# Attention output computed feature by token, its diagonals put into the score matrix

## The reference

```
for t in range(S):
    cur = einsum('bhd,bhe->bhde', u * k[t], v[t])
    y[t] = einsum('bhd,bhde->bhe', r[t], state + cur)
    state = w[:, None] * state + einsum('bhd,bhe->bhde', k[t], v[t])
```

## Time and profile before

| what | value |
|---|---|
| median of 3 runs | 1078.55 us (1077.47 to 1079.28) |
| the profiled execution | 1079.38 us |
| its span, first to last instruction | 1077.6 us |
| mean granted TensorE clock | 0.986 of full |
| TensorE busy, weight loads busy | 1039.0 us, 1030.1 us |
| VectorE, ScalarE, GpSimd busy | 819.8, 620.1, 446.8 us |

### The profile page before, as it was taken

How to read it: one execution, slowest core, us unless ns; L and a number is a source line. 1 busy time by engine, 2 the same in 40 slices (tenths; PEclk the granted TensorE clock), 3 DMA queues, 4 the chain that set the end, 5 groups by cost and what they waited for, 6 DMA issues and landing times.

```text
span 1077.6 us, 20183 instructions
## 1 busy us (share of the span) xinstructions
PE 1039.0 (96%) x6540; PEld 1030.1 (96%) x6540; DVE 819.8 (76%) x1998; ACT 620.1 (58%) x1477; POOL 446.8 (41%) x752
## 2 busy tenths in 40 slices
PE   5779899999999999999999999999999999999998
PEld 4779899999999999999999999999999999999998
DVE  8979888877778778778777534887786777687775
ACT  4334544343344343343343366888887888788886
POOL 7878767766666767767767044000000000000000
PEclk9779999999999999999999999999999999999999
DMA  3234422121121121122212123101000000000000
GB/s 110 90 124 126 125 67 75 52 74 53 52 77 52 53 75 52 53 74 61 70 63 70 56 95 118 59 23 45 23 23 23 22 22 23 23 0 22 1 23 23
DMA packets 22016, 61.15 MB, mean 57 GB/s; under 512 B 3104, under 2 KB 9376, under 8 KB 21920
## 3 DMA queue, kind: packets, MB, share of 16 engines
q1 hardware_dynamic: 19616, 50.55, 15.4%
q10 hardware_dynamic: 2304, 9.44, 2.2%
HBM read 50.54 MB, written 9.44 MB: 56 GB/s over the span
## 4 chain that ended last, share of the span: by engine, by line
PE 77%; DVE 9%; ACT 6%; issue 4%; DMA 2%; POOL 1%; ACTq 0%; DVEq 0%; SPq 0%; POOLq 0%
PE acc L1008 31%; PE hid L992 24%; PE lev_b L1037 5%; PE lev_a L1037 5%; PE tok L1059 3%; PE lev_b L992 3%; PE lev_a L992 3%; DMA w_raw<-weights 2%; ACT scratch L919 2%; ACT scratch L918 2%; DVE scratch L749 2%; DVE scores L545 1%; PE lev_b L1031 1%; PE tok L1054 1%; DVE scratch L742 1%
## 5 line engine op out<-in xcount | busy, mean ns | idle before, releaser
L1008 PE MATMUL acc<-g_hi,w_hi 128*128 128x384 f32 x768 | 268.9, 350 | 3.8 <-ACT result L834 3.8
L1008 PE MATMUL acc<-g_hi,w_lo 128*128 128x384 f32 x768 | 258.2, 336 | 0.0
L274 POOL TENSOR_TENSOR scratch<-rk_rows,power 48x128 f32<-48x128 f32 x528 | 239.6, 486 | 42.5 <-PE lev_a L1037 39.3
L992 PE MATMUL hid<-x_hi,w_hi 128*128 128x384 f32 x576 | 193.6, 336 | 3.6 <-DVE w_lo L658 1.6
L879 ACT ACTIVATE relu_neg<-hid 128x384 f32<-128x384 f32 x128 | 62.8, 490 | 231.7 <-PE hid L992 231.3
L992 PE MATMUL hid<-x_hi,w_lo 128*128 128x384 f32 x576 | 193.0, 335 | 0.0
L1008 PE MATMUL acc<-g_lo,w_hi 128*128 128x384 f32 x768 | 174.7, 335 | 0.1
L1008 PEld LDWEIGHTS acc<-g_hi,w_hi 128*128 128x128 f32 x768 | 145.0, 189 | 6.5 <-ACT result L834 4.8
L1008 PEld LDWEIGHTS acc<-g_hi,w_lo 128*128 128x128 f32 x768 | 145.0, 189 | 0.0
L1008 PEld LDWEIGHTS acc<-g_lo,w_hi 128*128 128x128 f32 x768 | 137.2, 188 | 0.7 <-DVE g_lo L767 0.6
L664 DVE SCALAR_TENSOR_TENSOR hid<-relu_neg,neg_slope,hid 128x384 f32<-128x384 f32 x128 | 79.3, 620 | 75.1 <-ACT hid L880 74.5
(11 more groups left out here) (110 smaller groups left out, 1987.8 us busy)
## 6 DMA issues: line engine op xcount, KB each, us to landing
rkv_tok<-rkv SPq DMA_DIRECT2D x24, 576.0 KB, 4.8
w_raw<-weights SPq DMA_DIRECT2D x32, 384.0 KB, 3.1
rk_rows<-rk_t SPq DMA_DIRECT2D x48, 192.0 KB, 3.3
prev<-rkv SPq DMA_DIRECT2D x48, 192.0 KB, 4.5
x_dram<-result ACTq DMA_DIRECT2D x8, 576.0 KB, 2.8
rkv_tok<-x_dram SPq DMA_DIRECT2D x8, 576.0 KB, 3.8
out<-result ACTq DMA_DIRECT2D x8, 576.0 KB, 2.8
bonus_tok<-bonus SPq DMA_DIRECT2D x1, 192.0 KB, 6.3
```

What stands on the lines that cost most here:

```text
L274: return engine.tensor_tensor(dst, src, spread(table[rows, pairs, 0:m], 2, CHUNK // (2 * m)), ALU.mult)
L992: last = nc.tensor.matmul(to[:, 0:TILE], w[:, j, kt * P:(kt + 1) * P], x[:, par, kt], start=x is x_hi and w is w_hi and kt == 0, stop=x is ...
L1008: last = nc.tensor.matmul(acc[d][:, 0:TILE], w[:, j, cols], g[:, j % RING], start=j == 0 and g is g_hi and w is w_hi, stop=j == STEPS - 1 ...
```

## The change

- `attend` swaps the sides: state and v are the stationary operands, the scaled r and `scores` the moving ones. The output has features on partitions (a head's 48 at partition 0 or 64) and tokens in columns, one block of 128 columns of the bank per pair. The state buffer has 112 columns for it. The transposes, y_tok and the four operations of the two outside terms are gone.
- The two outside terms go into `scores`: GpSimd makes the same products (the second now with the r of the following odd token, loaded into `r_next`), VectorE's `sum_diagonal` sums them and mixes them by even and odd tokens, and `fill_diagonal` (GpSimd, once per two pairs) writes both diagonals with a mask `places`, before ScalarE and VectorE put the levels in. `scores` has a buffer for every pair.
- x_hi and x_lo are 3 blocks of 128 partitions with the features of pairs 0 to 2 on 112 of them. Pair 3 is rounded and split into `y3`, and `fill_holes` moves it by six DMAs a chunk (16 partitions, hi and lo, 128 columns) into partitions 48 to 63 and 112 to 127 of the three blocks. The first weights' rows are put into that order on the host.
- Order: the products and the sums of a chunk are made one chunk ahead, x_hi and x_lo one step earlier (the fifth step). SyncE loads a chunk with `load_chunk`: the loads, then the six small DMAs of the chunk two before it, then `r_next`. Its loop now covers six chunks. The first `up` of a tile waits for all small DMAs of the tile. In step 0 of tile 1 the score comes before the `up`.

```diff
+        x_parts = sb("x_parts", [P, 2, 2, KT, TILE], F32R)
+        x_hi, x_lo = x_parts[:, :, 0], x_parts[:, :, 1]
         g_hi = sb("g_hi", [P, RING, TILE], F32R)
         g_lo = sb("g_lo", [P, RING, TILE], F32R)
         relu_neg = sb("relu_neg", [P, 2, TILE])
...
+        scores = sb("scores", [P, PAIRS, 2, CHUNK])
+        state = sb("state", [P, 2, PAIRS, ROWS])
+        y3 = sb("y3", [P, 2, CHUNK], F32R)
         power = sb("power", [P, PAIRS, CHUNK])
         power_rev = sb("power_rev", [P, PAIRS, CHUNK])
         power_tok = sb("power_tok", [P, PAIRS, 2, D])
@@ -121,10 +122,12 @@
...
 
@@ -276,34 +281,45 @@
 
         @block.sync
         def _(sp):
-            def load_prev(c, which, done):
...
+            def load_next(c):
+
+                if isinstance(c, int):
+                    reached(sp, s_sum, c)
+                odd = rkv[bass.ds(c, 1)].rearrange("c (i b) a f -> (c i) b a f", b=2)[:, 1, 0]
+                sp.dma_start(r_next[:], spread(odd, 1, 2)).then_inc(next_in, 16)
 
             def load_rows(c, par):
 
                 if isinstance(c, int):
-                    if c >= 2:
-                        sp.wait_ge(s_sum, c - 1)
-                        load_prev(c - 1, 0, prev_k_in)
-
                     reached(sp, score_done, PAIRS * (c - 1))
                     reached(sp, rstate_done, 2 * (c - 1))
...
                     sp.dma_start(rk_rows[HALF * q:HALF * q + D, par],
                                  rk_t[bass.ds(c, 1), q].rearrange("c d a p t -> (c d) a p t")
                                  ).then_inc(rows_in[par], 16)
                 if isinstance(c, int):
-                    reached(sp, y_done, c - 1)
+                    reached(sp, av_done, PAIRS * (c - 1))
+                    reached(sp, s_next, c - 1)
                 sp.dma_start(rkv_tok[:, par], rkv[bass.ds(c, 1)].rearrange("c t a f -> (c t) a f")
                              ).then_inc(tok_in[par], 16)
-                if not isinstance(c, int):
-                    load_prev(c - 1, 0, prev_k_in)
-                if not isinstance(c, int) or c >= 2:
-                    load_prev(c - 1, 1, prev_v_in)
+
+            def fill_holes(c, odd, cc):
+
+                sp.wait_ge(xlo_done, c + 1)
+                for q in range(2):
+                    for k in range(KT):
+                        first = HALF * q + (HALF - D) * k
+                        sp.dma_start(x_parts[HALF * q + D:HALF * (q + 1), odd, :, k, cc * CHUNK:(cc + 1) * CHUNK].bitcast(F32),
+                                     y3[first:first + HALF - D].bitcast(F32)).then_inc(holes_in, 16)
+
+            def load_chunk(c, at):
+
+                load_rows(c, at % 2)
+                before = at - 2
+                fill_holes(c - 2, before // CHUNKS_PER_TILE % 2, before % CHUNKS_PER_TILE)
+                load_next(c)
 
             def load_weights(i):
                 reached(sp, wlo_done, i - 1)
@@ -311,7 +327,8 @@
 
             def load_x2(u):
...
+            with sp.Fori(1, 3) as i:
+                for at in range(8, 8 + 2 * CHUNKS_PER_TILE):
+                    load_chunk(6 * i + at - 6, at)
+            for c in range(20, CHUNKS):
...
+            def products(c, par, uses):
+
+                pool.wait_ge(tok_in[par], 16 * uses)
+                reached(pool, s_sum, c)
+                nc.gpsimd.tensor_tensor(ruk[:], rkv_tok[:, par, 0], rkv_tok[:, par, 1], ALU.mult).then_inc(s_rk, 1)
+                pool.wait_ge(s_rk, c + 1)
+                if isinstance(c, int) and c == 0:
+                    pool.wait_ge(s_small, 32)
+                nc.gpsimd.tensor_tensor(ruk[:], ruk[:], bonus_tok[:], ALU.mult).then_inc(s_ruk, 1)
+                pool.wait_ge(next_in, 16 * (c + 1))
+                nc.gpsimd.tensor_tensor(r_next[:], r_next[:], rkv_tok[:, par, 1], ALU.mult).then_inc(s_next, 1)
+
+            def fill_diagonal(c, par, x):
 
                 pool.wait_ge(s_diag, c + 1)
-                nc.gpsimd.tensor_tensor(y_tok[:, par].rearrange("p (a d) -> p a d", d=D),
-                                        rkv_tok[:, par, 2].rearrange("p (a d) -> p a d", d=D),
-                                        spread(diag[:, par], 2, D), ALU.mult)
-                pool.wait_ge(prev_v_in, 16 * (c + 1))
-                nc.gpsimd.tensor_tensor(prev[:, 1].rearrange("p (a d) -> p a d", d=D),
-                                        prev[:, 1].rearrange("p (a d) -> p a d", d=D),
-                                        spread(diag_prev[:, par], 2, D), ALU.mult).then_inc(diagv_done, 1)
+                reached(pool, av_done, PAIRS * (c - 1) + 2 * x + 2)
+                heads = 2 * PAIRS // 2
+                dst = scores[:, 2 * x:2 * x + 2].rearrange("p a h (i b) -> p (a h) i b", b=2)
+                at = spread(places[:].rearrange("p (i b) -> p i b", b=2), 1, heads)
+                value = spread(diag[:, par, heads * x:heads * (x + 1)], 2, CHUNK // 2)
+                nc.gpsimd.tensor_tensor(dst, at, value, ALU.mult).then_inc(fill_done, 1)
...
+                products(c, par, uses)
+                scale_for_state(c, par, uses)
+                fill_diagonal(c, par, 0)
                 half_of_queries(c, par, 1, not first_tile)
-                pool.wait_ge(prev_k_in, 16 * (c + 1))
-                nc.gpsimd.tensor_tensor(prev[:, 0], rkv_tok[:, par, 0], prev[:, 0], ALU.mult).then_inc(s_prev, 1)
...
                 dve.wait_ge(score_done, w + 1)
                 dve.wait_ge(high_picked, picked_through(w, rep))
                 reached(dve, state_done, w - PAIRS + 1)
-                reached(dve, av_done, w - 1)
+                reached(dve, av_done, w - PAIRS + 1)
+                dve.wait_ge(fill_done, 2 * c + p // 2 + 1)
 
                 for q in range(2):
-                    rows, cols = slice(HALF * q, HALF * q + D), slice(D * q, D * q + D)
...
@@ -550,35 +578,29 @@
             def sum_diagonal(c, par):
 
                 dve.wait_ge(s_ruk, c + 1)
-                reached(dve, diagv_done, c - 1)
-                nc.vector.tensor_reduce(diag[:, par], y_tok[:, par].rearrange("p (a d) -> p a d", d=D),
-                                        AXIS.X, ALU.add)
-                dve.wait_ge(s_prev, c + 1)
-                nc.vector.tensor_reduce(diag_prev[:, par], prev[:, 0].rearrange("p (a d) -> p a d", d=D),
+                reached(dve, fill_done, 2 * c - 2)
+                nc.vector.tensor_reduce(diag[:, par, :, 0], ruk[:].rearrange("p (a d) -> p a d", d=D),
+                                        AXIS.X, ALU.add).then_inc(s_mix, 1)
+                dve.wait_ge(s_next, c + 1)
+                nc.vector.tensor_reduce(diag_next[:], r_next[:].rearrange("p (a d) -> p a d", d=D),
                                         AXIS.X, ALU.add).then_inc(s_sum, 1)
+                dve.wait_ge(s_mix, 2 * c + 1)
+                nc.vector.tensor_scalar(diag[:, par, :, 1], diag[:, par, :, 0], odd_token[:, 0:1], None, ALU.mult
+                                        ).then_inc(s_mix, 1)
+                dve.wait_ge(s_mix, 2 * c + 2)
                 dve.wait_ge(s_sum, c + 1)
-                nc.vector.tensor_scalar(diag_prev[:, par], diag_prev[:, par], odd_token[:, 0:1], None, ALU.mult
-                                        ).then_inc(s_diag, 1)
-
-            def add_terms(c, par):
-
-                dve.wait_ge(diagv_done, c + 1)
-                nc.vector.tensor_tensor(y_tok[:, par], y_tok[:, par], prev[:, 1], ALU.add).then_inc(term_done, 1)
-
-            def add_diagonal(c, par, bank):
-
-                dve.wait_ge(term_done, c + 1)
-                dve.wait_ge(av_done, 4 * c + 4)
-                nc.vector.tensor_tensor(y_tok[:, par], bank[:, 0:FEATURES], y_tok[:, par], ALU.add
-                                        ).then_inc(y_done, 1)
+                nc.vector.scalar_tensor_tensor(diag[:, par, :, 1], diag_next[:], even_token[:, 0:1],
+                                               diag[:, par, :, 1], ALU.mult, ALU.add).then_inc(s_diag, 1)
...
-                nc.vector.tensor_tensor(x_lo[:, odd, :, columns],
-                                        bank[:, 0:FEATURES].rearrange("p (k n) -> p k n", k=KT),
-                                        x_hi[:, odd, :, columns].bitcast(F32), ALU.subtract).then_inc(xlo_done, 1)
+                nc.vector.tensor_tensor(y3[0:ROWS, 1], bank[0:ROWS, third:third + CHUNK],
+                                        y3[0:ROWS, 0].bitcast(F32), ALU.subtract)
+                nc.vector.tensor_tensor(x_lo[0:ROWS, odd, :, columns],
+                                        bank[0:ROWS, 0:third].rearrange("p (k n) -> p k n", k=KT),
+                                        x_hi[0:ROWS, odd, :, columns].bitcast(F32), ALU.subtract).then_inc(xlo_done, 1)
...
+                    last_of_chunk = rep < TILES and ends_chunk(j)
+                    following = cc + 1 < CHUNKS_PER_TILE or more
+                    opens = rep == 1 and j == 0
+                    if not opens:
+                        activate(s, j)
```

(30 more changed lines are left out.)

201 lines of the change are left out of this document (94 added, 107 removed).

## The result

The changed kernel takes 1131.34 us (median of 4 runs, 1128.66 to 1132.08), the kernel before 1078.01 in the same session: a ratio of 1.0492, 95% interval 1.0468 to 1.0516. Forecast were 1104.5 and a range of 1069 to 1126. The sign was right, the size half of what came.

The account below looks back on a forecast made before the run. TensorE was taken to bound the kernel, never resting from 151.9 to 614.7 us. Transposes -7.1, passes 0, turnovers +20, edges +11, start and tile 1 +2 gave +26 us on 1078.55: 1104.5 us, range 1069 to 1126.

Parts of the forecast that it names:

- transposes: TensorE, 21 chunks in 7 tiles: three transposes per chunk go, 0.34 us each chunk, -7.1 us.
- attend's passes: TensorE's six passes per attend stay six at unchanged cost: 0, or -9 us if two heads' passes overlap by one.
- turnovers: TensorE going to part-array products and back in each attend: 0.24 us by 84, +20 us; ends 0 and 0.70 each.
- edges, rest: TensorE waits for six small DMAs at each tile's start: about 2.0 us at five edges, 0.5 at two, +11 us.
- edges, clock: Half clock for 3 us after each edge's rest, 1.5 us an edge, 9 us: counted in the upper end only.
- Start and tile 1: First tile and tile 1: less VectorE work against a later first copy, DMA waits and turnovers; +2 us, ends -4 and +8.
- costed at nothing: Added work on GpSimd, VectorE and SyncE, and four score buffers instead of two, taken to cost or save nothing.
- A: The forecast itself: turnovers cost 0.12 to 0.36 us an attend, edges 1 to 2.5 us; range 1090 to 1117; chance 0.41.
- B: Rival: turnovers cost nothing, edges stay; +7 to -2 us, about 1081 us; chance 0.26.
- C: Rival, faster: free turnovers, heads overlap by one pass, small DMAs land before TensorE asks; about 1070 us; chance 0.15.
- D: Rival: turnovers fully bare, 0.5 to 0.7 us by 84 attends, +42 to +59 us; 1127 to 1143 us; chance 0.15.
- E: Rival: GpSimd's score fill becomes the limit and ScalarE waits for it at chunk starts; 1100 us; chance 0.03.

Follow-up runs that it names:

- g_same: Changed kernel with both heads' products of an attend on the same weight columns and output rows, so they cannot lie side by side; 1142.13 us, ratio 1.0576.
- f_full: Changed kernel with both products of an attend made 96 weight columns wide, so none uses part of the array (output mixed); 1123.87 us, ratio 1.0410.
- l_order: k_holes_first with SyncE's order of loads, weights and small transfers in the first tile written anew; 1086.14 us, ratio 1.0070.
- n_nodiag: Changed kernel without small transfers, chunk 1's product loads behind the first weights, scores filled from the bonus row instead of the sums; 1088.30 us, ratio 1.0083.
- i_both: Changed kernel with half the small transfers on ScalarE's queue from the second tile on, and diagonal sums behind x_lo; 1112.30 us, ratio 1.0313.
- k_holes_first: i_both with SyncE's small transfers ahead of the row and token loads of the chunk after next, from the second tile on; 1102.43 us, ratio 1.0223.
- e_sum: Changed kernel with the next chunk's diagonal sums one step later on VectorE, behind x_lo; 1117.69 us, ratio 1.0360.
- p_state_first: l_order with GpSimd scaling the state's keys ahead of the diagonal products and VectorE making chunk 0's sums two pieces earlier; 1091.01 us, ratio 1.0119.

## Why the prediction was wrong

**The size failed, by two terms**, the first tile (20 us too low) and the edges (22 us too low); the attend's terms were 10 us too high and hid part of it. By the sum's own steps:

| term | forecast | came | from |
|---|---|---|---|
| transposes | -7.1 | -7 | steps that had them, 5.02 to 4.67 us |
| attend's passes | 0 (to -9) | -18 | 0.21 of overlap by 84 (g_same) |
| turnovers | +20 (0.24 each) | +28 | 0.33 by 84 (g_same less f_full) |
| edges, rest | +11 | +21 | 22.1 less 1.3 of wait |
| edges, clock | 0 (9 in the upper end) | +12 | 7 first steps, together 12 longer |
| first tile and tile 1 | +2 | +22 in the first tile | 66.8 to 88.5 |

That is 58 for 52.7 measured. Tiles 2 to 7 come out within 0.5 us of their terms (30.6 us measured). Tile 1, which had waits of its own before, is 1.5 us under its terms, and the part without attention nearly 3; why is open.

**Start and tile 1 is the step whose mechanism failed**: +2 us forecast, +22 came in the first tile alone. I listed for the first tile what each engine does more, and found the first copy 1.6 us late. I hadn't walked SyncE's queue through it. The step says that SyncE is "costed at nothing", on counts of issue time, and that behind the small transfers stand "only the next chunk's loads and r_next". True from tile 2 on; in the first tile weights 1 to 3 and the product loads of chunks 2 and 3 stand there, behind a wait for x_lo, and nothing runs ahead to cover it. l_order shows it: same work, another order of that queue, 16.7 us less. Of the 5 us that are left I have no split; n_nodiag puts about 1 on the chain of the sums, as an estimate.

**Edges: the mechanism held, its price was a third of the real one** (11 us forecast, 33 came). x_lo came 1.7 us ahead of TensorE's want (forecast 1.5). Then I took 0.35 us from issue to issue, from the loads, and it is 0.64; that is 1.5 us later for the last of six, about the whole difference between the 2.0 forecast and the 3.4 that came. The kernel before had the higher price too: the step costed at nothing has its prev loads at 0.54 to issue, and I gave no reason for taking the lower one. Landing was 1.8 (forecast 1.5). rkv_tok was not what bound: it landed at 421.5, two us before the last of them. The loads bind once the issues are quicker (i_both), which k_holes_first shows by putting the transfers ahead. Two edges were set down at 0.5 us and cost more: the one at tile 4, where I let the old wait of 1.3 us cover most of the new one, rested 4.8, so nothing was covered; the last rested 1.9. And the clock: because 1.34 us of rest had left it full I kept half clock for the upper end. All seven rests, of 1.9 to 4.8 us, were followed by 3.4 us of it or more.

**The attend: half of what was forecast, by two errors against each other.** The turnovers cost 0.33 us, inside the ends of 0 and 0.70 and above the 0.24 taken. The overlap, of which I had allowed one pass in the lower end, is two passes: all four lie side by side in pairs. The net is 0.11, not 0.24, and +9 us instead of +20. That this error brought the forecast nearer to the measured time was luck: with the attend right and the rest as it was, it would have missed by 10 us more. The Trainium skill, "TensorEngine Tiling (Array Packing)", Key Properties, has a change of mode drain the TensorE; that it costs time is borne out by g_same less f_full, which gives the price.

**Of the rivals**, A's mechanisms were those at work from tile 2 on; its own range ended 14 us too low. B's turnovers at no cost are refuted by f_full and g_same, and so are C's; C's overlap of the heads is there, and is larger than it said. D had 0.5 to 0.7 bare: 0.33 was measured. E doesn't occur from tile 2 on: TensorE waits there for x_parts alone.

**What would show it**: attends spaced 1.1 us forecast, 0.95 came, between A and B; edges of 2 us, 2.8 to 3.2 came at five and 4.8 and 1.9 at the others; steps without transposes as said; first copy at 17.5, 21.8 came, and that one line, ended by a DMA of the weights, shows the failed step.

## What to carry to other kernels

Where a change puts an entry that waits into a queue of DMA issues, write that queue out in order, for the start of the kernel as well as for its steady state, with the time at which each entry becomes ready; what an engine has more to do says little of it. Moving one late entry may show nothing, because the next takes its place: test the whole order at once. Small transfers that a saturated engine waits for went best ahead of large prefetches, both in the queue and in time (k_holes_first, 10 us).

## What the chip showed that I had not expected

- A transfer of 16 KB from SBUF to SBUF took 0.59 us to issue on SyncE, with 0.64 from one to the next, and on ScalarE about the same (three in 1.90), where the loads of rk_rows and rkv_tok took mostly 0.32 to 0.42. It isn't the source in SBUF that sets this: the loads of r_next took 0.58 to 0.65 as well.
- Such transfers landed 1.8 to 2.1 us after issue with no load ahead of them (k_holes_first), 2.8, 2.4 and 2.2 us while rkv_tok was still landing (the first three of the changed kernel's edge), and 4.2 to 4.6 behind 960 KB of loads issued in the 1.5 us before (i_both).
- Two products of 48 weight columns on rows 0 and 64 of the output, in float32 with its two passes each, ran side by side and gave 0.21 us per attend; going to such products and back cost 0.33, of which 0.20 on the way back.
- A rest of 3.2 us at an edge was followed by 3.4 us at 1.2 GHz, the one of 0.30 us in k_holes_first by none. In between the length of the rest doesn't decide: one of 1.9 us was followed by half clock in the changed kernel and two in e_sum, while others of 1.9 and 2.5 us in e_sum, 2.9 in g_same and 3.2 in p_state_first were not.
- In l_order the second step of tile 4, where the loops start over, took 8.62 us instead of 5.24: ScalarE stood 3.35 us and VectorE 3.75 for nothing that the profile shows. The kernel before has its one wait, 1.3 us, at the start of this tile as well, and the changed kernel its longest, 4.8. What it is stays open.
